# An attention block and two MLPs on one core: the first tile's inverse taken on 128x4 sums, dummy products ahead of the keys, and four edits of order and buffers

## The reference

```python
kv_pool = kv.reshape(B, H // 4, 4, W // 4, 4, C).mean(axis=(2, 4))      # 768 keys of 128
k = v = kv_pool.reshape(B, -1, C) @ w_sr
s = (q @ k.T) / sqrt(C);  s = s - s.max(-1)                             # q: 12288 x 128
a = exp(s);  a /= a.sum(-1) + 1e-09;  x = a @ v
h = x @ w_in;   x = where(h >= 1, h, where(h <= -1, 0, (h + 1)**2 / 4)) @ w_out    # 128 -> 2048 -> 128
h = x @ w_in2;  y = (h / (1 + exp(-1.702 * h))) @ w_out2                           # 128 -> 2048 -> 128
```

## Time and profile before

| | us |
|---|---|
| median of 3 runs | 1320.02 (1318.38 to 1321.22) |
| profiled execution, time | 1320.54 |
| profiled execution, span | 1318.7 |
| busy: PE / POOL / ACT / DVE | 1274.6 / 1145.5 / 1007.7 / 1002.1 |
| chain that ended last, by engine | PE 82%, POOL 7%, issue 6%, DVE 3% |

### The profile page before, as it was taken

The page is one execution under the profiler, slowest core; times in us unless marked ns, Lnnn a source line. Parts: engine busy times, 40 slices in busy tenths (PEclk is TensorE's granted clock), DMA queues, the critical chain, the costliest instruction groups (busy, mean ns, idle before and its releaser), DMA issues.

```text
span 1318.7 us, 16960 instructions
## 1 busy us (share of the span) xinstructions
PE 1274.6 (97%) x5468; PEld 1028.7 (78%) x5468; DVE 1002.1 (76%) x1146; ACT 1007.7 (76%) x1070; POOL 1145.5 (87%) x477
## 2 busy tenths in 40 slices
PE   4888999999999999999999999999999999999988
PEld 3446888888888888888888888888888888878866
DVE  6878779779788787797787887877978878756433
ACT  2567788887878887878778788878788787886756
POOL 2337999999999999999999999999999999998760
PEclk9998999999999999999999999999999999999999
DMA  9000000000010010000000000100000000000000
GB/s 347 22 17 24 17 17 32 16 17 17 16 32 16 16 32 16 16 31 17 16 16 16 32 16 16 32 16 16 28 20 16 16 17 25 9 17 17 1 8 17
DMA packets 18258, 35.72 MB, mean 27 GB/s; under 512 B 3248, under 2 KB 3376, under 8 KB 17968
## 3 DMA queue, kind: packets, MB, share of 16 engines
q1 hardware_dynamic: 18224, 35.30, 8.2%
HBM read 28.90 MB, written 6.39 MB: 27 GB/s over the span
## 4 chain that ended last, share of the span: by engine, by line
PE 82%; POOL 7%; issue 6%; DVE 3%; ACT 1%; DMA 1%; SPq 0%; POOLq 0%; ACTq 0%; DVEq 0%
PE ps_ring L449 16%; PE ps_ring L450 15%; PE ps_ring L451 15%; PE ps_y L449 11%; PE ps_y L451 11%; PE ps_y L450 11%; POOL g_lo L367 5%; POOL pt_lo L367 2%; DMA kv_sb<-in_kv_t 1%; PE ps_y L527 1%; PE ps_y L552 1%; DVE g L979 0%; DVE s_third L926 0%; DVE part_max L865 0%; DVE g_hi L970 0%
## 5 line engine op out<-in xcount | busy, mean ns | idle before, releaser
L367 POOL TENSOR_TENSOR g_lo<-g,g_hi 128x1024 fp32r<-128x1024 f32 x365 | 930.1, 2578 | 92.1 <-DVE g L979 86.7
L970 DVE SCALAR_TENSOR_TENSOR g_hi<-g,ps_ring 128x1024 fp32r<-128x1024 f32 x184 | 224.1, 1218 | 151.6 <-ACT g L768 150.7
L749 ACT ACTIVATE g<-ps_ring 128x1024 f32<-128x1024 f32 x192 | 197.2, 1027 | 182.8 <-PE ps_ring L451 178.6
L449 PE MATMUL ps_y<-g_hi,w_hi 128*128 128x512 f32 x752 | 297.0, 395 | 11.8 <-DVE y_lo L824 7.0
L450 PE MATMUL ps_y<-g_lo,w_hi 128*128 128x512 f32 x752 | 293.7, 391 | 0.0
L451 PE MATMUL ps_y<-g_hi,w_lo 128*128 128x512 f32 x752 | 293.7, 391 | 0.0
L979 DVE SCALAR_TENSOR_TENSOR g<-g,ps_ring 128x1024 f32<-128x1024 f32 x192 | 233.0, 1213 | 9.6 <-ACT g L768 9.6
L761 ACT ACTIVATE g<-ps_ring 128x1024 f32<-128x1024 f32 x192 | 197.9, 1031 | 17.0 <-PE ps_ring L451 10.4
L768 ACT ACTIVATE g<-g 128x1024 f32<-128x1024 f32 x192 | 204.2, 1063 | 5.4
L751 ACT ACTIVATE g_hi<-ps_ring 128x1024 fp32r<-128x1024 f32 x192 | 195.9, 1020 | 5.1 <-PE ps_y L451 5.1
L449 PEld LDWEIGHTS ps_y<-g_hi,w_hi 128*128 128x128 f32 x752 | 141.4, 188 | 49.7 <-POOL g_lo L367 10.6
(11 more groups left out here) (114 smaller groups left out, 1675.4 us busy)
## 6 DMA issues: line engine op xcount, KB each, us to landing
kv_sb<-in_kv_t SPq DMA_DIRECT2D x12, 512.0 KB, 8.6
q_sb<-in_q_t SPq DMA_DIRECT2D x24, 256.0 KB, 3.6
out_t<-y_sb SPq DMA_DIRECT2D x24, 256.0 KB, 3.6
key_max<-max_row SPq DMA_DIRECT2D x23, 256.0 KB, 3.4
inv_sum<-inv_row SPq DMA_DIRECT2D x23, 256.0 KB, 3.3
w_raw<-in_moe_w_in SPq DMA_DIRECT2D x2, 1024.0 KB, 17.7
max_row<-max_turned SPq DMA_DIRECT2D x23, 2.0 KB, 1.3
inv_row<-inv_turned SPq DMA_DIRECT2D x23, 2.0 KB, 1.3
```

The costliest lines, as they stand in the source:

```text
L367: return nc.gpsimd.tensor_tensor(dst, src, upper.bitcast(F32), ALU.subtract)
L449: nc.tensor.matmul(dst, l_hi, r_hi, start=start, stop=False)
L749: nc.scalar.activation(g2[:, slot, :], ps_h2(k), ACT.Gelu_apprx_sigmoid).then_inc(g2_done, 1)
L970: nc.vector.scalar_tensor_tensor(out=g1_hi[:, uu % 2, :], in0=g1[:, uu % 2, :], scalar=1.0, in1=ps_h1(k), op0=ALU.min, op1=ALU.max).then_i ...
```

## The change

- POOL's set-up: `ident` becomes 128x128, `minus_ones` is made from `ones`, `spare` goes.
- TensorE: after each of window groups 4 to 7, two float32 products of 256 columns into an unused bank (eight in all), ahead of `project_k(0)`. `project_k(1)` comes after three score chunks instead of four. The lower part of the first keys is made in two halves, each with its own wait.
- DVE: chunk 0 of tile 0 gets its maximum alone; `k_lower` comes after it, then chunk 1 alone.
- ACT no longer makes the upper part of `w_in1`; POOL does, half by half, the second half after `max_masked` has come to 2.
- The first tile's sums: four products with `key_sums` as the stationary operand and one column of `ones` (128x4 sums, a query's sum on its own partition), DVE inverts 128x4 and multiplies an identity by it, one product with `ones` turns and spreads it, ACT copies it to `inv_sum`, and the first unit of the first MLP starts with `x_hi` and takes `x_lo` last.
- Stage of tile 3 on DVE: the three maxima ahead of the steps, one shift a step, the last `add_keys` of tile 2 a step later.
- Iteration 24: the lower parts of tile 23's probabilities go from POOL to DVE.
- Iterations 26 and 27: the turns of the ring are counted on; TensorE's wait there is for the block it takes.

```diff
+        def ring_turn(it, k):
+            return k + U * (it - NT - 1) if blockless(it) else k
+
+        def ps_h2(it, k):
+            return ps_ring[:, (2 + 2 * ring_turn(it, k)) % 3, :]
+
+        def ps_h1(it, k):
+            return ps_ring[:, (3 + 2 * ring_turn(it, k)) % 3, :]
...
+        def blockless(it):
+            return isinstance(it, int) and it >= NT + 2
...
             def iteration(it, half):
-                if is_tile(it - 1):
+                if is_tile(it - 1) and not is_number(it, NT):
                     for p in range(PAIRS):
                         probs_lower(it - 1, 1 - half, p)
...
-            lower(k_lo[:, 0:FIRST_KEYS], k_sb[:, :], k_hi[:, 0:FIRST_KEYS]).then_inc(k_lo_first, 1)
+            for b in range(2):
+                keys = slice(b * FIRST_KEYS // 2, (b + 1) * FIRST_KEYS // 2)
+                lower(k_lo[:, keys], k_sb[:, keys], k_hi[:, keys]).then_inc(k_lo_first, 1)
             q_lower(1, q1_lo[:, :], q_sb[:, 1, :], q1_hi[:, :])
+            w_upper(0, 0)
             w_lower(0, 0)
+            pool.wait_ge(max_masked, 2)
+            w_upper(0, 1)
             w_lower(0, 1)
...
-            def spread_sums():
+            def sum_first_keys():
                 pe.wait_ge(s_early, KC)
                 pe.wait_ge(keys_added, 5)
-                nc.tensor.matmul(ps_y2[:, :], ones[:, :], key_sums[:, 4, :], start=True,
+                for j in range(QUADS):
+                    last = nc.tensor.matmul(ps_y2[:, j:j + 1], key_sums[:, 4, j * P:(j + 1) * P], ones[:, 0:1],
+                                            start=True, stop=True)
+                last.then_inc(first_summed, 1)
+
+            def spread_inverse():
+                pe.wait_ge(inverse_masked, 1)
+                nc.tensor.matmul(ps_y2[:, :], ones[:, :], key_sums[:, 0, :], start=True,
                                  stop=True).then_inc(sums_spread, 1)
...
-                if c % 2 == 0:
+                if c % 2 == 0 and is_number(t, NT - 1):
+                    pe.wait_ge(pt_lo_last, c // 2 + 1)
+                elif c % 2 == 0:
                     pe.wait_ge(pt_lo_done, (t - WHOLE) * PAIRS + (c // 2 + 1))
...
+            def first_unit(dst):
+                pe.wait_ge(w_lo_done[0], 1)
+                pe.wait_ge(x_hi_done, 1)
+                for d in range(2):
+                    f = slice(d * P, (d + 1) * P)
+                    half = dst[:, d * T:(d + 1) * T]
+                    nc.tensor.matmul(half, w_hi[:, f], x_hi[:, 0, :], start=True, stop=False)
+                    nc.tensor.matmul(half, w_lo[:, f], x_hi[:, 0, :], start=False, stop=False)
+                pe.wait_ge(x_lo_done, 1)
+                for d in range(2):
+                    f = slice(d * P, (d + 1) * P)
+                    last = nc.tensor.matmul(dst[:, d * T:(d + 1) * T], w_hi[:, f], x_lo[:, 0, :], start=False, stop=True)
+                last.then_inc(h1_ready, 1)
...
-                    if not layer1 or (k == 1 and not is_tile(it - 2)):
+                    if not layer1:
                         at_least(pe, g2_hi_done, n - 1)
-                    if k == 0:
-                        at_least(pe, g1_done, it * U - 18 if unit(it, k - 1, FIRST1)[0] else NT * U)
+                    if blockless(it):
+                        pe.wait_ge(g1_done, min(it * U + k - 19, NT * U))
+                    elif k == 0:
+                        at_least(pe, g1_done, it * U - 18)
...
             pe.wait_ge(w_scaled, 2)
+            for g in range(4, FIRST_GROUPS):
+                pe.wait_ge(summed, g)
+                for _ in range(2):
+                    nc.tensor.matmul(ps_k[:, 3, 0:4 * GK], w_k[:, :], window_sum[:, 0:4 * GK], start=True, stop=True)
             project_k(0)
             project_v(0)
-            for c in range(FIRST_CHUNKS):
+            for c in range(FIRST_CHUNKS - 1):
                 score_chunk(0, c)
             project_k(1)
+            score_chunk(0, FIRST_CHUNKS - 1)
             project_v(1)
...
             for c in range(4):
                 value_chunk(0, c)
-            spread_sums()
-            for c in range(4, KC):
-                value_chunk(0, c)
+            sum_first_keys()
+            value_chunk(0, 4)
+            spread_inverse()
+            value_chunk(0, 5)
...
-            w_upper(0)
             evacuate(1, 1)
             for p in range(PAIRS):
                 exponential_first(p)
+            act.wait_ge(sums_spread, 1)
+            copy(inv_sum[:, :], ps_y2[:, :]).then_inc(inverse_copied, 1)
...
+            def invert_first():
+                dve.wait_ge(first_summed, 1)
+                nc.vector.tensor_scalar(inv_first[:, :], ps_y2[:, 0:QUADS], 1e-9, None, ALU.add).then_inc(first_eps, 1)
+                dve.wait_ge(first_eps, 1)
+                nc.vector.reciprocal(inv_first[:, :], inv_first[:, :]).then_inc(first_inverse, 1)
+                dve.wait_ge(first_inverse, 1)
+                nc.vector.tensor_tensor(key_sums[:, 0, :].rearrange("p (j i) -> p j i", i=P),
+                                        ident[:, :].unsqueeze(1).to_broadcast([P, QUADS, P]),
+                                        inv_first[:, :].unsqueeze(2).to_broadcast([P, QUADS, P]),
+                                        ALU.mult).then_inc(inverse_masked, 1)
+
             def normalise_first():
-                dve.wait_ge(sums_spread, 1)
-                nc.vector.tensor_scalar(inv_sum[:, :], ps_y2[:, :], 1e-9, None, ALU.add).then_inc(eps_added, 1)
-                dve.wait_ge(eps_added, 1)
-                nc.vector.reciprocal(inv_sum[:, :], inv_sum[:, :]).then_inc(inverted, 1)
-                dve.wait_ge(inverted, 1)
+                dve.wait_ge(inverse_copied, 1)
                 dve.wait_ge(pv_done, KC)
...
                 if is_tile(it - 2):
                     normalise(it - 2)
+                if is_number(it, NT):
+                    for p in range(PAIRS):
+                        last_probs_lower(it - 1, 1 - half, p)
...
+            first_chunk_maximum()
+            k_lower()
             maximum(0, 0, 0)
-            k_lower()
...
             add_first_keys()
+            invert_first()
             maximum(1, 1, 2)
             normalise_first()
...
+            for p in range(PAIRS):
+                maximum(3, 1, p)
             for k in range(U):
...
                 if k == 0:
-                    maximum(3, 1, 0)
-                    maximum(3, 1, 1)
+                    shift(2, 0, 0)
                 if k == 1:
-                    shift(2, 0, 0)
-                    maximum(3, 1, 2)
+                    shift(2, 0, 1)
+                    fold_maximum(3)
                 if k == 2:
-                    shift(2, 0, 1)
                     shift(2, 0, 2)
-                    fold_maximum(3)
                 if k == 4:
                     add_keys(2, 0, 0)
                     add_keys(2, 0, 1)
+                if k == 5:
                     add_keys(2, 0, 2)
-                if k == 5:
                     invert(2)
```

More of the change, by code:

```diff
@@ L85, in encoder_kernel @@
             minus_ones = sb(ramp, "minus_ones", [P, P], F32R)
-            ident = sb(ramp, "ident", [P, SQ])
-            spare = sb(ramp, "spare", [P, P])
+            inv_first = sb(ramp, "inv_first", [P, QUADS])
+            ident = sb(ramp, "ident", [P, P])
         pt_hi = sb(ctx, "pt_hi", [P, KC, T], F32R)
@@ L220, in encoder_kernel @@
         pt_lo_done = sem("pt_lo_done")
+        pt_lo_last = sem("pt_lo_last")
         pv_done = sem("pv_done")
@@ L359, in _ @@
             nc.gpsimd.memset(ident[:, :], 0.0).then_inc(cleared, 1)
-            nc.gpsimd.memset(spare[:, :], -1.0).then_inc(cleared, 1)
-            pool.wait_ge(cleared, 2)
+            pool.wait_ge(cleared, 1)
             nc.gpsimd.affine_select(out=ident[:, :], in_=ident[:, :], compare_op=ALU.not_equal, fill=1.0,
-                                    base=0, pattern=[[-1, SQ]], channel_multiplier=1).then_inc(ident_ready, 1)
-            nc.gpsimd.tensor_copy(minus_ones[:, :], spare[:, :]).then_inc(ones_ready, 1)
+                                    base=0, pattern=[[-1, P]], channel_multiplier=1).then_inc(ident_ready, 1)
+            pool.wait_ge(ones_ready, 1)
+            nc.gpsimd.tensor_scalar(minus_ones[:, :], ones[:, :], -1.0, None, ALU.mult).then_inc(ones_ready, 1)
             def lower(dst, src, upper):
@@ L371, in q_lower, with w_upper @@
                 lower(dst, src, upper).then_inc(q_lo_done, 1)
-            def w_upper(m):
+            def w_upper(m, p):
                 pool.wait_ge(w_loaded[m], 16)
-                for p in range(WP):
-                    cols = slice((m * WP + p) * WCH, (m * WP + p + 1) * WCH)
-                    nc.gpsimd.tensor_copy(w_hi[:, cols], w_raw[:, cols]).then_inc(w_hi_done[m], 1)
+                cols = slice((m * WP + p) * WCH, (m * WP + p + 1) * WCH)
+                nc.gpsimd.tensor_copy(w_hi[:, cols], w_raw[:, cols]).then_inc(w_hi_done[m], 1)
             def w_lower(m, p):
@@ L471, in score_chunk @@
```

(26 more changed lines are left out.)

52 lines of the change are left out of this document (34 added, 18 removed).

## The result

| | before | after |
|---|---|---|
| median, us | 1319.41 (4 runs, 1318.38 to 1321.22) | 1302.26 (4 runs, 1301.22 to 1303.24) |
| ratio, 95% interval | | 0.9868 [0.9851, 0.9886] |
| profiled execution: time / span | 1320.54 / 1318.7 | 1302.89 / 1301.1 |
| chain that ended last | PE 82%, POOL 7%, issue 6% | PE 89%, POOL 5%, issue 3% |

A forecast was written before the change was run, and what follows sets the result against it. TensorE, without idle from 300 to 1150 us, was taken as the bound, so only its waits and slow stretches at the ends could be won: 7.1 + 3.0 + 2.9 + 5.9 = 18.9 off 1320.54, stated as 1301.5, range 1298.0 to 1306.5.

The forecast's parts named there:

- A: Start of the kernel, up to unit 0's out product: 7.1 us less; low end 2.8, high end 7.7.
- The fall "to 2.8": Start: if the dummy products don't bring the clock up and it stays low until 25, only 2.8 us are won.
- The four lengths: Start: TensorE's work before its clock rose, 8.6, 4.2, 3.8 and 3.1 us in the earlier trace; 4.0 was taken.
- B: Stage of tile 3, wait before unit 8's out product: 3.0 us less, POOL's `g_lo` becoming last; 2.0 to 3.9.
- The other reading: Stage of tile 3: DVE and POOL slow each other in proportion, so one shift less gives back some 0.4, making 3.4.
- the 2.0 us of idle that follow take it: Stage of tile 3: the moved `add_keys` makes tile 3's shifts 1.16 us later, absorbed by DVE's following idle.
- C: Iteration 24: TensorE's wait for POOL and nine slow products go, 2.9 us less after later waits; 2.0 to 3.9.
- D: Iterations 26 and 27: two ring waits and seven slow products go, 0.7 given back on POOL: 5.9 us less; 4.0 to 6.6.
- The loop, 0: Loop's body: unchanged in effect, so nothing won or lost.
- the rivals: Low clock 1305.8 (0.13), end pays part 1304.4 (0.13), better 1297.5 (0.06), slower loop 1327 (0.03), new waits 1308 to 1315 (0.03).
- rival 1: Start: the float32 dummies don't bring the clock up before the scores; gain there only 2.8, time 1305.8; chance 0.13.

The follow-up runs named there:

- experiment 3: Kernel before with only DVE's three maxima of tile 3 ahead of its units, one shift a step, the last `add_keys` a step later: 1315.87 us, ratio 0.9976.
- experiment 6: Changed kernel with 16 extra products that keep TensorE busy in the wait at unit 8: 1304.03 us, ratio 0.9884.
- experiment 5: Changed kernel unaltered, measured once more: 1302.50 us, ratio 0.9873.
- 2: Kernel before with only the lower parts of tile 23's probabilities moved from POOL to DVE: 1316.67 us, ratio 0.9981.
- 8: Kernel before with only the eight dummy products ahead of the keys added: 1317.25 us, ratio 0.9986.
- experiment 1: Kernel before with only the turns of the ring counted on in iterations 26 and 27: 1312.58 us, ratio 0.995.
- experiment 12: Changed kernel with unit 191's lower part on DVE and the very last unit's lower part in two separately awaited halves: 1301.68 us, ratio 0.9866.

## Why the prediction was right

1301.5 was forecast and 1302.26 measured, inside the range; it was faster by far more than 0.2%. The waits that were to go went, and those that were to take their place came. That the sum is so close is in part luck: the profile of the kernel before holds slow clock stretches that other executions of the same code don't have, and two terms of nothing (0.78 won, 1.0 lost) nearly cancel.

- **A, 7.1:** 6.8 at unit 0's mark in this pair of traces. The four profiles with the old start have 53.41 to 55.12 there and the seven with the new one 47.26 to 48.28, so that it could have been 5.1 or 7.9; the averages are 6.6 apart. By difference of the medians it is 5.4; 0.4 of what is lacking shows at unit 8, which in the changed kernel comes 45.4 us behind the mark and not the 44.95 of experiment 3. The terms were right (float32 dummies bring the clock up before the keys, the inverse 1.9 at its place, the subtraction bound by TensorE). Two sizes were off. The fall "to 2.8" without a risen clock, that is 4.3 for the dummies, measured 1.2 to 1.5 and 2.5: it took the 24.95 of the earlier trace rows as the time at which the clock rises by itself, and in two of five kernels without dummies it had risen by 21.3 or 21.6. The inverse won 1.9 at its place and 1.2 in the median. The four lengths from which the 4.0 us were taken leave out a fifth of the same trace, the 5.2 us from 101.95 to 107.14.
- **B, 3.0:** 2.5 at the wait, 3.0 there when alone (experiment 3), 3.1 in that run's median. The 0.78 behind it is a draw: from the out product of unit 8 to the first product behind the slow stretch it is 4.4 to 5.3 us over all profiles but that of experiment 6. A wait took another's place, as said, and POOL's `g_lo` took 3.29 there for the 3.26 of the earlier trace rows: it waits for the shift. The other reading, by which one shift less would have won 0.4, falls. The Trainium skill (SBUF — State Buffer, "Who interferes with whom") says that of a two-input DVE instruction and a GpSimd one the later waits until the earlier is over; this row agrees. One step was wrong: the moved `add_keys` was put at nothing, since "the 2.0 us of idle that follow take it". They did not, and TensorE stands 0.5 for DVE in the scores of tile 4 (experiment 5).
- **C, 2.9:** 2.9, and 2.3 alone. Some 1.6 of it is the slow stretch, which the code of before doesn't have in every execution (experiment 3). The three lower parts took 4.21 on DVE for the 3.7 forecast, and were hidden.
- **D, 5.9:** 5.7, and 6.4 alone, with the 0.7 for POOL given back where it was said. Here too some 1.5 is a slow stretch, which 2 and 8 don't have.
- **The loop, 0:** it took back 1.0 in the first profile, with the wait at tile 4 in it; by nine profiles it is 0.5 on average, 0.3 of it that wait.

Of the rivals none came. The doubt of rival 1, whether float32 products raise the clock, is answered: they do, as dummies and as projections. In experiment 1 the projections are all that TensorE ran before its first score product, and that one has the full clock already.

## What to carry to other kernels

Price a slow clock stretch by several executions: one profile shows one draw, and here the same code ran its first scores at either clock. When the longest wait of a stretch is cut, look for the wait behind it on every engine of the chain first: keeping TensorE busy, or taking 2 us off POOL, gained nothing in the median where POOL's or DVE's next instruction was as late. An engine's idle time that is to take a moved instruction should be checked against everything that moves with it: 2.0 us were not enough for a moved 1.2 here, since another instruction grew by 0.8. In the last two iterations no later wait took the gain back: 0.5 and 1.0 us stayed whole in the trace of experiment 12.

## What was not expected of the hardware

- Idle of 2.02 to 2.08 us brought a slow stretch of seven or eight products in three profiles (before, experiments 3 and 6) and none in two others (1, 8); 2.35 brought one in two (before, 3) and none in two (2, 8); 2.44 in none of four (before, 2, 3, 8); 3.27 to 7.05 in all, six to fourteen products long.
- With the same start the eight dummy products took 5.2 to 5.6 us in some profiles and 6.2 to 6.5 in others, and unit 0's mark lies between 47.26 and 48.28: a scatter of 1 us from the first 20 us alone. The Trainium skill (TensorE: Matmul & The Clock Gate, "What's actually happening") says that the clock's watch isn't aligned to the start of the kernel; this agrees.
